# A fused attention, convolution and expert kernel: attention updates placed behind the next scores, and four smaller moves

## The chip, the cores and the metric

The kernel runs on one core of one Trainium2 chip. A core has a matrix engine (TensorE, PE in the profile), a vector engine (VectorE, DVE), a scalar engine (ScalarE, ACT), a general engine (GpSimd, POOL) and a queue engine (SyncE, SP) that here only issues transfers. Each engine works through its own list of instructions in order and waits on semaphores for the others. The metric is the device time of one execution in microseconds; lower is better.

## The reference

Three layers in a row, everything in float32. The core of it:

```python
# 1: decayed linear attention, B=2, H=8 heads, S=768, D=64; gamma differs per head
for t in range(S):
    state = gamma * state + einsum('bhd,bhe->bhde', k[:, :, t], v[:, :, t])
    y[:, :, t] = scale * einsum('bhd,bhde->bhe', q[:, :, t], state)
# 2: x = y as (2, 768, 512);  w_in 512x1024, conv_w 3x1024, w_out 1024x512
h = maximum(x @ w_in, 0)
conv_out = sum of conv_w[k] * (h shifted by k - 1 in the sequence), k = 0..2
x = (h * sigmoid(conv_out)) @ w_out
# 3: 8 experts, w1 512x1024, w2 1024x512
logits = x @ w_gate;  local_gate = sigmoid(x @ w_local)
e = argmax(logits[s]) if s == 0 or local_gate[s] < 0.5 else the expert of s - 1
out[s] = softmax(logits[s])[e] * (maximum(x[s] @ w1[e], 0) @ w2[e])
```

## The kernel before

**Precision.** Products that must be exact are made of three: a float32 matrix is split into a high part (a cast by ScalarE) and a low part (the value less its high part, by VectorE or GpSimd), and `three` (L961 to L963) multiplies high by low, low by high and high by high.

**Attention.** The 16 heads of both batches are taken as 8 pairs, i = 0 to 7. A pair's sequence is cut into 6 chunks of 128, in two halves g = 0, 1 of three chunks. For each pair TensorE makes: `scores(i, g)` (L991, keys times queries within chunks), `updates(i)` (L975, what each chunk adds to the state, into one bank), and `values(i, g)` (L1012 masked scores times values, L1009 scaled queries times state). VectorE makes `mask(i, g)` (scores times decay, L711), `scan(i)` (the states of all chunks from the updates, L697) and `y_lo(i, g)` (low part of the result, L718). ScalarE scales the keys that the updates read (`k_scale`, L531), two pairs ahead, and copies the results' high parts (L543). GpSimd scales the queries (L410). SyncE loads queries and keys for the scores (`qk`, 768 KB a pair), keys and values in rows (`kv`, 2 x 384 KB) and the decay tables (192 KB for each of the four pairs of heads). There are four buffers each for `qk` and `kv`; pair i + 4 is loaded once the values of pair i are done (`pv_done`). Behind them SyncE loads w_in in four pieces and, last, the output weights transposed and straight (2 MB each).

The weights of the input projection are split while the last pairs run: ScalarE casts four pieces (L547), GpSimd makes their four low parts (`lo`, L396). The convolution stage then starts with a gate product (`gate_first`, L1040, reads the transposed output weights), and its projection takes the four pieces one after another in its first sweep.

**Experts.** Tokens are sorted by expert into blocks of 128 (17 here, each of one expert). A block's rows are gathered from DRAM (`x2_rows`) by an indirect transfer from GpSimd, turned by TensorE (`turn_x`, L1214), split into `xT` high (ScalarE L625) and low (VectorE L891), multiplied by W1 (`through_w1`), passed through ReLU (ScalarE L620), turned (`turn_h`, L1262), split into `hT` high (L632) and low (L899) and multiplied by W2 (`through_w2`). VectorE scales the result (`evac_out`, L905), and GpSimd scatters it to the output (`scatter`, L449). An expert's weights come in 4 pieces of 128x1024 for W1 and 4 for W2; ScalarE casts each (L570), and the low parts are split between VectorE (L882) and GpSimd (L426). TensorE runs one block's W1 ahead of the previous block's W2.

Block 0 is special: its xT is made in two halves (ScalarE L650, VectorE L922), partly from rows that are still in SBUF. Block 1 is the first that needs `x2_rows` whole, with its last tile, which ScalarE writes in two halves (L648). Where a high and a low part are named in a list as `weights_lo(w, e, slot, pieces)`, w is 0 for W1 and 1 for W2, and e the expert.

The order on each engine is that of the code; no scheduler changes it.

## Time and profile before

| | us |
|---|---|
| median of 3 runs | 433.14 |
| lowest, highest | 432.61, 433.22 |
| the profiled execution | 432.46 |
| its span (first to last instruction) | 430.7 |
| TensorE busy in it | 413.1 |
| VectorE, ScalarE, GpSimd busy | 223.1, 196.0, 149.6 |

The profile is of one execution. Busy times are sums over instructions, and an engine that is not on the path may be idle without cost. In rows in order of time the first number is the start, the second the duration of the group in us, and the bracket at the end says how long the engine had been idle before it and whom it waited for.

### The profile page before, as it was taken

To read this page: it belongs to the slowest core of one execution; us is meant where nothing else is said; L and a number is where in the kernel's file an instruction comes from. 1 tells how busy PE (TensorE), PEld (TensorE's weight loads), DVE (VectorE), ACT (ScalarE), POOL (GpSimd) and SP (SyncE) were. 2 spreads that over 40 slices of the span, in tenths; PEclk is the share of its full clock that TensorE was granted. 3 is DMA by queue.
4 is the path that set the end of the run, shared out by engine and by line. 5 is a ranking of instruction groups with operands and counts; after the bars stand their busy time and mean duration, and the time that the engine had idled before them with its cause. 6 is when DMAs were issued, how large, how long until landed. Compare 5 with 4: busy or idle time off the path is not lost.

```text
span 430.7 us, 7239 instructions
## 1 busy us (share of the span) xinstructions
PE 413.1 (96%) x2641; PEld 349.0 (81%) x2642; DVE 223.1 (52%) x290; ACT 196.0 (46%) x276; POOL 149.6 (35%) x125
## 2 busy tenths in 40 slices
PE   7699999999999999999889999999999999999992
PEld 4588889987889987779778888888888888888862
DVE  4478837875002879389785422117642461726340
ACT  2244566862114666280435522128751472827440
POOL 3440884000000000015562821124882282653661
PEclk9999999999999999999999999999999999999997
DMA  8989900000321006742149391110479108366110
GB/s 299 414 336 372 420 22 2 0 2 0 148 97 49 2 0 258 328 148 97 50 157 419 132 410 52 49 50 24 173 278 414 67 25 330 128 229 235 36 33 9
DMA packets 15578, 67.77 MB, mean 157 GB/s; under 512 B 2559, under 2 KB 3583, under 8 KB 11200
## 3 DMA queue, kind: packets, MB, share of 16 engines
q1 hardware_dynamic: 12352, 58.88, 34.8%
q0 software_dynamic: 2912, 8.13, 5.8%
q8 instruction: 17, 0.28, 0.3%
q10 hardware_dynamic: 288, 0.41, 0.3%
q14 instruction: 9, 0.07, 0.1%
HBM read 58.49 MB, written 10.22 MB: 160 GB/s over the span
## 4 chain that ended last, share of the span: by engine, by line
PE 84%; DMA 5%; DVE 4%; ACT 2%; POOL 2%; SPq 1%; issue 1%; POOLq 0%; DVEq 0%
PE ps L961 24%; PE ps L963 23%; PE ps L962 23%; DMA kv<-qkv 5%; DVE wx L882 3%; PE ps L1262 3%; PE ps L1214 2%; PE ps L1012 1%; PE ps L1062 1%; PE ps L1009 1%; PE ps L991 1%; ACT wx L570 1%; POOL wx L426 1%; PE ps L975 1%; PE ps L1071 1%
## 5 line engine op out<-in xcount | busy, mean ns | idle before, releaser
L426 POOL TENSOR_TENSOR wx<-raw_w,wx 128x1024 fp32r<-128x1024 f32 x21 | 53.5, 2563 | 14.7 <-ACT wx L570 14.6
L961 PE MATMUL ps<-wx,xT 128*128 128x512 f32 x136 | 54.7, 402 | 2.4 <-DVE xT L891 1.5
L570 ACT CAST wx<-raw_w 128x1024 fp32r<-128x1024 f32 x56 | 54.8, 1057 | 1.9 <-issue 1.3
L961 PE MATMUL ps<-wx,hT 128*128 128x512 f32 x136 | 54.6, 401 | 0.7 <-POOL wx L426 0.7
L963 PE MATMUL ps<-wx,hT 128*128 128x512 f32 x136 | 53.1, 391 | 0.0
L963 PE MATMUL ps<-wx,xT 128*128 128x512 f32 x136 | 53.1, 391 | 0.0
L962 PE MATMUL ps<-wx,xT 128*128 128x512 f32 x136 | 53.0, 389 | 0.0
L962 PE MATMUL ps<-wx,hT 128*128 128x512 f32 x136 | 52.9, 389 | 0.0
L882 DVE TENSOR_TENSOR wx<-raw_w,wx 128x1024 fp32r<-128x1024 f32 x35 | 48.0, 1419 | 4.8 <-ACT wx L570 4.0
L632 ACT CAST hT<-ps 128x512 fp32r<-128x512 f32 x34 | 18.3, 590 | 57.1 <-PE ps L1262 57.1
L470 POOL TENSOR_TENSOR bk<-ge 128x240 f32<-128x240 f32 x1 | 0.6, 587 | 123.0 <-DVE ge L843 123.0
L961 PE MATMUL ps<-x,win 128*128 128x384 f32 x128 | 43.2, 337 | 0.0
L963 PE MATMUL ps<-x,win 128*128 128x384 f32 x128 | 42.8, 334 | 0.0
L962 PE MATMUL ps<-x,win 128*128 128x384 f32 x128 | 42.8, 334 | 0.0
L905 DVE TENSOR_SCALAR os<-ps,pslot 128x512 f32<-128x512 f32 x17 | 12.8, 751 | 57.1 <-PE ps L963 52.1
L620 ACT ACTIVATE hs<-ps 128x512 f32<-128x512 f32 x34 | 20.1, 597 | 46.1 <-PE ps L963 46.1
L961 PE MATMUL ps<-wout,hg 128*128 128x512 f32 (+1 forms) x104 | 40.1, 386 | 0.0
L891 DVE TENSOR_TENSOR xT<-ps,xT 128x512 fp32r<-128x512 f32 x17 | 11.7, 691 | 54.1 <-ACT xT L625 54.1
L962 PE MATMUL ps<-wout,hg 128*128 128x512 f32 (+1 forms) x104 | 38.9, 374 | 0.0
L963 PE MATMUL ps<-wout,hg 128*128 128x512 f32 (+1 forms) x104 | 38.9, 374 | 0.0
L750 DVE SCALAR_TENSOR_TENSOR cv<-hpad,cvw,cv 128x768 f32<-128x768 f32 x16 | 16.9, 1058 | 40.7 <-ACT cv L586 40.5
L449 POOL DMA_INDIRECT out<-os,snow x17 | 18.2, 1069 | 44.5 <-DVE os L905 32.9
(162 smaller groups left out, 813.3 us busy)
## 6 DMA issues: line engine op xcount, KB each, us to landing
raw_w<-w_exp SPq DMA_DIRECT2D x28, 1024.0 KB, 8.7
qk<-qkv SPq DMA_DIRECT2D x7, 768.0 KB, 7.4
...
```

The costliest lines, as they stand in the source:

```text
L426: ins = nc.gpsimd.tensor_tensor(wx[:, slot, 1, c], raw, wx[:, slot, 0, c].bitcast(F32), ALU.subtract)
L449: nc.gpsimd.indirect_dma_start(out_rows, bass.IndirectOffsetOnAxis(snow[:, 0:1], 0), os_[:], None, bounds_check=T - 1, oob_is_err=False).t ...
L570: nc.scalar.copy(wx[:, slot, 0, c], raw).then_inc(wx_hi[w], 1)
L620: nc.scalar.activation(hs[:, 512 * a:512 * a + 512], psP1[:, 512 * a:512 * a + 512], ACT.Relu).then_inc(h_done, 1)
L632: nc.scalar.copy(hT[:, 0, 4 * a:4 * a + 4, :].rearrange("p k t -> p (k t)"), psHT[:, 512 * a:512 * a + 512]).then_inc(hT_hi, 1)
L750: nc.vector.scalar_tensor_tensor(c[:], hp[:, 0:S], cvw[:, f, 0:1], c[:], ALU.mult, ALU.add).then_inc(tap0, 1)
L882: ins = nc.vector.tensor_tensor(wx[:, slot, 1, c], raw, wx[:, slot, 0, c].bitcast(F32), ALU.subtract)
L905: nc.vector.tensor_scalar(os_[:], psO, pslot[:, bass.ds(g, 1)], None, ALU.mult).then_inc(o_done, 1)
L961: mm(o, lh, rl, start=first, stop=False)
L962: mm(o, ll, rh, start=False, stop=False)
L963: return mm(o, lh, rh, start=False, stop=last)
L1262: last = nc.tensor.transpose(psHT[:, P * k:P * k + P], hs[:, P * k:P * k + P], ident)
```

## The change

Names and places are those of the code above.

- SyncE: pairs 1 to 3 are loaded alike, `qk`, keys, values, and each pair's decay table by itself: for pair 1 ahead of the values as before, for pairs 2 and 3 behind them. Keys and values of pairs 2 and 3 are two transfers now, with a semaphore each. The decay tables of pairs 2 and 3 were one transfer ahead of pair 2's `kv`.
- TensorE: `updates(i + 1)` stands between `scores(i + 1, 0)` and `values(i, 1)` for all pairs; it stood ahead of `values(i, 0)` for all but the first.
- ScalarE: `k_scale(i + 2)` follows the two copies of pair i; it preceded them. VectorE: `mask(i, 0)` precedes `scan(i)`.
- GpSimd: the low parts of w_in start one pair later: part 0 behind the scaling of pair 6, parts 1 to 3 behind that of pair 7.
- The last tile's rows are stored in two halves. GpSimd copies block 1's index before it waits for the stores, not after.
- VectorE at the start of the experts: first half of xT ahead of W2's piece 3; pieces 1 and 2 of expert 1's W1 behind block 0's hT.
- The last product waits for the four low parts of the last W2 in steps: VectorE's two at its start, GpSimd's ahead of its fifth and seventh groups; 4 filler matmuls ahead of it instead of 8. The last scatter's index is copied ahead of the wait for VectorE's result, which has a semaphore of its own.

```diff
@@ -325,21 +327,21 @@
             sp.dma_start(kv[0][:, 1, :], qkv[0, :, 3, :]).then_inc(kv_in[0], 16)
             sp.dma_start(decay[:, 0], decay_c[:, 0]).then_inc(decay0_in, 16)
             sp.dma_start(qk[0][:, :, HALF:S], qkv[0, :, 0:2, HALF:S]).then_inc(qk_in[0], 16)
-            sp.dma_start(qk[1][:], qkv[1, :, 0:2, :]).then_inc(qk_in[1], 16)
-            sp.dma_start(kv[1][:, 0, :], qkv[1, :, 2, :]).then_inc(k1_in, 16)
-            sp.dma_start(decay[:, 1], decay_c[:, 1]).then_inc(decay1_in, 16)
-            sp.dma_start(kv[1][:, 1, :], qkv[1, :, 3, :]).then_inc(kv_in[1], 16)
-            for i in range(2, B * NP_):
+            for i in range(1, NP_):
+                sp.dma_start(qk[i][:], qkv[i, :, 0:2, :]).then_inc(qk_in[i], 16)
+                sp.dma_start(kv[i][:, 0, :], qkv[i, :, 2, :]).then_inc(k_in[i], 16)
+                if i == 1:
+                    sp.dma_start(decay[:, i], decay_c[:, i]).then_inc(decay_in[i], 16)
+                sp.dma_start(kv[i][:, 1, :], qkv[i, :, 3, :]).then_inc(kv_in[i], 16)
+                if i > 1:
+                    sp.dma_start(decay[:, i], decay_c[:, i]).then_inc(decay_in[i], 16)
+            for i in range(NP_, B * NP_):
                 j = i % 4
-                if i >= 4:
-                    sp.wait_ge(pv_done, 2 * (i - 4) + 2)
+                sp.wait_ge(pv_done, 2 * (i - 4) + 2)
                 sp.dma_start(qk[j][:], qkv[i, :, 0:2, :]).then_inc(qk_in[j], 16)
-                if i == 2:
-                    sp.dma_start(decay[:, 2:], decay_c[:, 2:]).then_inc(decay_in, 16)
                 sp.dma_start(kv[j][:], qkv[i, :, 2:4, :]).then_inc(kv_in[j], 16)
-                if i >= 4:
-                    c = slice(1024 * (i - 4), 1024 * (i - 4) + 1024)
-                    sp.dma_start(win_raw[:, c], w_in[:, c]).then_inc(win_in[i - 4], 16)
+                c = slice(1024 * (i - 4), 1024 * (i - 4) + 1024)
+                sp.dma_start(win_raw[:, c], w_in[:, c]).then_inc(win_in[i - 4], 16)
                 if i == 5:
                     sp.dma_start(con[:], const_c).then_inc(const_in, 16)
             sp.dma_start(cvw[:], conv_w).then_inc(small_in, 16)
@@ -362,10 +364,16 @@
...
-                sp.wait_ge(x2_out, t + 1 if t < TT - 1 else TT + 1)
+                if t == TT - 1:
+                    break
+                sp.wait_ge(x2_out, t + 1)
                 if t < TT - 2:
                     sp.dma_start(x2_early[t * P:(t + 1) * P, :], x2n[:, t % 3, :]).then_inc(x2_stored[t % 3], 16)
                 sp.dma_start(x2_rows[t * P:(t + 1) * P, :], x2n[:, t % 3, :]).then_inc(x2_stored[t % 3], 16)
+            for n in range(2):
+                h = slice(DM // 2 * n, DM // 2 * n + DM // 2)
+                sp.wait_ge(x2_out, TT + n)
+                sp.dma_start(x2_rows[T - P:T, h], x2n[:, (TT - 1) % 3, h]).then_inc(x2_stored[(TT - 1) % 3], 16)
@@ -401,18 +409,15 @@
...
-                    pool.wait_ge(decay0_in, 16)
-                if i == 1:
-                    pool.wait_ge(decay1_in, 16)
-                if i == 2:
-                    pool.wait_ge(decay_in, 16)
+                if i < NP_:
+                    pool.wait_ge(decay_in[i], 16)
...
-                if i >= 5:
-                    lo(win, win_raw, i - 5)
-            for n in range(3, 4):
+                if i >= 6:
+                    lo(win, win_raw, i - 6)
+            for n in range(2, 4):
                 lo(win, win_raw, n)
@@ -426,7 +431,7 @@
...
-                        ins.then_inc(w2_last_lo if is_last(e) else w2_lo, 1)
+                        ins.then_inc(w2_last_lo_pool if is_last(e) else w2_lo, 1)
@@ -485,10 +490,15 @@
                 bounds_check=T - 2 * P - 1, oob_is_err=False).then_inc(gathered, 16)
             weights_lo(0, 0, 0, (3,))
             weights_lo(1, 0, 0, (0,))
+            pool.wait_ge(gathered, 16)
+            pool.wait_ge(xg_free, 2)
+            nc.gpsimd.tensor_copy(gnow[:], gidx[:, 1:2]).then_inc(g_copied, 1)
+            pool.wait_ge(g_copied, 2)
+            pool.sem_inc(rows_known, 1)
             for j in range(3):
-                pool.wait_ge(x2_stored[j], 32 * (TT // 3) - 16 * (j > 0))
-            pool.wait_ge(gathered, 16)
-            gather(1)
+                pool.wait_ge(x2_stored[j], 32 * (TT // 3) - 16 * (j == 1))
+            nc.gpsimd.indirect_dma_start(
+                xg[:], None, x2_rows, bass.IndirectOffsetOnAxis(gnow[:, 0:1], 0)).then_inc(gathered, 16)
             weights_lo(1, 0, 0, (1,))
@@ -510,7 +520,14 @@
             weights_lo(1, E - 1, 1, (2, 3))
             scatter(last)
             last = plain(E - 1)
-            scatter(last)
+            pool.wait_ge(scattered, 16 * last + 16)
+            nc.gpsimd.tensor_copy(snow[:], sidx[:, bass.ds(last, 1)]).then_inc(s_copied, 1)
+            pool.wait_ge(s_copied, last + 1)
+            pool.sem_inc(rows_known, 1)
+            pool.wait_ge(o_last, 1)
+            nc.gpsimd.indirect_dma_start(
+                out_rows, bass.IndirectOffsetOnAxis(snow[:, 0:1], 0), os_[:], None,
+                bounds_check=T - 1, oob_is_err=False).then_inc(scattered, 16)
             pool.wait_ge(gathered, 16 * last + 48)
             pool.wait_ge(scattered, 16 * last + 32)
@@ -525,7 +542,7 @@
...
-                act.wait_ge(k0_in if i == 0 else k1_in if i == 1 else kv_in[j], 16 * (i // 4 + 1))
+                act.wait_ge(k_in[i] if i < 4 else kv_in[j], 16 * (i // 4 + 1))
@@ -535,12 +552,12 @@
             k_scale(1)
             for i in range(B * NP_):
                 b, p = i // NP_, i % NP_
-                if i + 2 < B * NP_:
-                    k_scale(i + 2)
                 for g in range(2):
                     n, tb = 2 * i + g, S * b + HALF * g
                     act.wait_ge(pv_done, n + 1)
                     nc.scalar.copy(x1[:, 0, p, tb:tb + HALF], psY[n % 3]).then_inc(yhi_done, 1)
+                if i + 2 < B * NP_:
+                    k_scale(i + 2)
                 for n in {4: (0,), 5: (1, 2), 6: (3,)}.get(i, ()):
@@ -722,8 +736,8 @@
             scan(0)
             mask(0, 1)
             for i in range(1, B * NP_):
+                mask(i, 0)
                 scan(i)
-                mask(i, 0)
                 y_lo(i - 1, 0)
                 mask(i, 1)
                 y_lo(i - 1, 1)
@@ -899,10 +913,10 @@
...
+            def evac_out(g, done):
                 dve.wait_ge(p2_done, g + 1)
                 dve.wait_ge(scattered, 16 * g + 16)
-                nc.vector.tensor_scalar(os_[:], psO, pslot[:, bass.ds(g, 1)], None, ALU.mult).then_inc(o_done, 1)
+                nc.vector.tensor_scalar(os_[:], psO, pslot[:, bass.ds(g, 1)], None, ALU.mult).then_inc(done, 1)
@@ -910,22 +924,23 @@
...
             dve.wait_ge(tables, 1)
             weights_lo(0, 0, 0, (0, 1, 2))
-            weights_lo(1, 0, 0, (3,))
             for n in range(2):
+                if n == 1:
+                    weights_lo(1, 0, 0, (3,))
                 dve.wait_ge(x0_hi if n == 0 else xT_hi, 1)
                 nc.vector.tensor_tensor(xT[:, 1, 2 * n:2 * n + 2], psX0[:, 2 * n:2 * n + 2],
                                         xT[:, 0, 2 * n:2 * n + 2].bitcast(F32),
                                         ALU.subtract).then_inc(x0_lo if n == 0 else xT_done, 1)
-            weights_lo(0, 1, 1, (0, 1), True)
+            weights_lo(0, 1, 1, (0,), True)
             x_lo(1)
             h_lo(0)
-            weights_lo(0, 1, 1, (2,))
+            weights_lo(0, 1, 1, (1, 2))
...
             h_lo(last + 1)
             last = plain(E - 1)
-            evac_out(last)
+            evac_out(last, o_last)
@@ -967,7 +982,7 @@
                 pe.wait_ge(k_scaled, 2 * i + 2)
                 if i:
                     pe.wait_ge(st_done, 2 * i)
-                if i < 2:
+                if i < 4:
                     pe.wait_ge(kv_in[i], 16)
@@ -1020,13 +1035,10 @@
             warm_up(2, psY[2])
             pe.wait_ge(zeroed, 2)
             for i in range(B * NP_):
-                if 0 < i and i + 1 < B * NP_:
-                    updates(i + 1)
                 values(i, 0)
                 if i + 1 < B * NP_:
                     scores(i + 1, 0)
-                if i == 0:
-                    updates(1)
+                    updates(i + 1)
                 values(i, 1)
                 if i + 1 < B * NP_:
                     scores(i + 1, 1)
@@ -1241,11 +1253,13 @@
 
             def through_w2(g, e, slot):
                 if is_last(e):
-                    pe.wait_ge(w2_last_lo, 4)
+                    pe.wait_ge(w2_last_lo, 2)
                 else:
                     pe.wait_ge(w2_lo, 4 * e + 4)
                 pe.wait_ge(o_done, g + 1)
                 for k in range(KF):
+                    if is_last(e) and k in (4, 6):
+                        pe.wait_ge(w2_last_lo_pool, k // 2 - 1)
                     if k % 4 == 0:
                         pe.wait_ge(hT_done, 2 * g + k // 4 + 1)
@@ -1305,7 +1319,7 @@
             pe.wait_ge(w1_lo_dve, E)
             step(last_block, E - 2, 0, 1)
             last_block = plain(E - 1, 1)
-            warm_up(8, bank(7))
+            warm_up(4, bank(7))
             through_w2(last_block, E - 1, 1)
```

TensorE around pair 2's updates. In the rows kv_63 is pair 2's keys and values, kv_62 pair 1's, qk_59 pair 2's queries and keys; L975 are updates, L1009 and L1012 values, L991 scores. Before:

```order
L975 MATMUL ps<-kv_63 64x64 [waits st_done,k_scaled]
L975 MATMUL ps<-kv_63 64x64 x9
L1012 MATMUL ps<-probs_69,kv_62 64x128 [waits masked,q_scaled]
L1012 MATMUL ps<-probs_69,kv_62 64x128
L1009 MATMUL ps<-qs_66,state_72 64x128 [waits st_done]
L1009 MATMUL ps<-qs_66,state_72 64x128
L1012 MATMUL ps<-probs_69,kv_62 64x128 x2
L1009 MATMUL ps<-qs_66,state_72 64x128 x2
L1012 MATMUL ps<-probs_69,kv_62 64x128 x2
L991 MATMUL ps<-qk_59 128x128 [waits masked,qk_in2]
L991 MATMUL ps<-qk_59 128x128 x5
```

The same place now (L990 updates, L1024 and L1027 values, L1006 scores):

```order
L1027 MATMUL ps<-probs_69,kv_62 64x128 [waits masked,q_scaled]
L1027 MATMUL ps<-probs_69,kv_62 64x128
L1024 MATMUL ps<-qs_66,state_72 64x128 [waits st_done]
L1024 MATMUL ps<-qs_66,state_72 64x128
L1027 MATMUL ps<-probs_69,kv_62 64x128 x2
L1024 MATMUL ps<-qs_66,state_72 64x128 x2
L1027 MATMUL ps<-probs_69,kv_62 64x128 x2
L1006 MATMUL ps<-qk_59 128x128 [waits masked,qk_in2]
L1006 MATMUL ps<-qk_59 128x128 x5
L990 MATMUL ps<-kv_63 64x64 [waits kv_in2,st_done,k_scaled]
L990 MATMUL ps<-kv_63 64x64 x9
```

The updates that wait for pair 2's keys stood ahead of pair 1's first values and pair 2's first scores, and stand behind both now.

VectorE at the start of the experts, from W2's piece 3 (raw_first_94) and the two halves of block 0's xT (128x256) to block 0's hT; raw_w_1_96 is expert 1's W1. Before:

```order
L882 TENSOR_TENSOR wx<-raw_first_93,wx 128x1024 [waits wx_hi0] x2
L882 TENSOR_TENSOR wx<-raw_first_94,wx 128x1024 [waits wx_hi1]
L922 TENSOR_TENSOR xT<-ps,xT 128x256 [waits x0_hi]
L922 TENSOR_TENSOR xT<-ps,xT 128x256 [waits xT_hi]
L882 TENSOR_TENSOR wx<-raw_w_1_96,wx 128x1024 [waits wx_hi0] x2
L891 TENSOR_TENSOR xT<-ps,xT 128x512 [waits xT_hi]
L899 TENSOR_TENSOR hT<-ps,hT 128x512 [waits hT_hi] x2
L882 TENSOR_TENSOR wx<-raw_w_1_96,wx 128x1024 [waits wx_hi0]
```

Now (L896 weights, L937 and L905 xT, L913 hT):

```order
L896 TENSOR_TENSOR wx<-raw_first_93,wx 128x1024 [waits wx_hi0] x2
L937 TENSOR_TENSOR xT<-ps,xT 128x256 [waits x0_hi]
L896 TENSOR_TENSOR wx<-raw_first_94,wx 128x1024 [waits wx_hi1]
L937 TENSOR_TENSOR xT<-ps,xT 128x256 [waits xT_hi]
L896 TENSOR_TENSOR wx<-raw_w_1_96,wx 128x1024 [waits wx_hi0]
L905 TENSOR_TENSOR xT<-ps,xT 128x512 [waits xT_hi]
L913 TENSOR_TENSOR hT<-ps,hT 128x512 [waits hT_hi] x2
L896 TENSOR_TENSOR wx<-raw_w_1_96,wx 128x1024 [waits wx_hi0] x2
```

The first half of xT went ahead of W2's piece 3, and one of two pieces of expert 1's W1 went behind block 0's hT.

GpSimd at the same place, the second gather. Before:

```order
L426 TENSOR_TENSOR wx<-raw_first_93,wx 128x1024 [waits wx_hi0]
L426 TENSOR_TENSOR wx<-raw_first_94,wx 128x1024 [waits wx_hi1]
L436 CAST gnow<-gidx 128x1 [waits gathered,x2_stored2,xg_free,x2_stored1,x2_stored0]
L439 DMA xg<-x_rows,gnow 128x512 [waits g_copied]
L426 TENSOR_TENSOR wx<-raw_first_94,wx 128x1024 [waits wx_hi1]
L436 CAST gnow<-gidx 128x1 [waits xg_free,gathered,tables]
```

Now (L431 weights, L495 and L500 the second gather):

```order
L431 TENSOR_TENSOR wx<-raw_first_93,wx 128x1024 [waits wx_hi0]
L431 TENSOR_TENSOR wx<-raw_first_94,wx 128x1024 [waits wx_hi1]
L495 CAST gnow<-gidx 128x1 [waits xg_free,gathered]
L500 DMA xg<-x_rows,gnow 128x512 [waits g_copied,x2_stored2,x2_stored1,x2_stored0]
L431 TENSOR_TENSOR wx<-raw_first_94,wx 128x1024 [waits wx_hi1]
L441 CAST gnow<-gidx 128x1 [waits xg_free,gathered,tables]
```

The index copy no longer waits for the stores (x2_stored); the transfer behind it does.

## Rows read from the trace of the kernel before

**Rows 1.** The page, part 1: busy us (share of the span) xinstructions.

```profile
PE 413.1 (96%) x2641; PEld 349.0 (81%) x2642; DVE 223.1 (52%) x290; ACT 196.0 (46%) x276; POOL 149.6 (35%) x125
```

**Rows 2.** TensorE in order of time: start us, us, line, operation [wait <-for whom].

```profile
14.85 0.94 PE L991 MATMUL ps<-qk 64*128 64x128 f32 x12
...
19.63 1.19 PE L975 MATMUL ps<-kv 128*64 128x64 f32 x20 [3.85 <-ACT kv L531]
...
23.92 0.50 PE L1009 MATMUL ps<-qs,state 128*64 128x128 f32 x4
...
26.32 0.80 PE L975 MATMUL ps<-kv 128*64 128x64 f32 x20
...
31.43 0.80 PE L975 MATMUL ps<-kv 128*64 128x64 f32 x20
...
54.66 1.92 PE L1040 MATMUL ps<-woutT,wgl 128*32 128x512 f32 x16
```

**Rows 3.** Stretches: us; busy us of PE, PEld, DVE, ACT, POOL; PEclk, DMA share, GB/s.

```profile
20.00:23.00 3.00, 3.00 (x38) 2.67 (x34) 2.97 (x5) 1.09 (x3) 1.83 (x1) 0.50 1.02 418
28.00:33.00 5.00, 5.00 (x91) 4.43 (x88) 4.27 (x7) 2.08 (x4) 1.81 (x1) 1.00 1.03 419
25.20:27.40 2.20, 2.20 (x48) 1.91 (x46) 1.28 (x3) 1.54 (x3) 0.78 (x1) 1.00 0.42 95
```

**Rows 4.** ScalarE in order of time, attention.

```profile
18.46 1.12 ACT L531 ACTIVATE kv<-kv,con 128x384 f32<-128x384 f32 x2 [6.18 <-DMA kv<-qkv]
...
44.94 1.12 ACT L531 ACTIVATE kv<-kv,con 128x384 f32<-128x384 f32 x2 [2.60 <-DMA kv<-qkv]
```

**Rows 5.** The load queue (SyncE) in order of time: the issue after pair 1.

```profile
25.55 0.33 SPq L336 DMA_DIRECT2D qk<-qkv  x1
```

**Rows 6.** GpSimd in order of time, end of the attention.

```profile
50.14 1.82 POOL L410 TENSOR_TENSOR qs<-qk,decay 128x768 f32<-128x768 f32 x1
51.93 4.72 POOL L396 TENSOR_TENSOR win<-win_raw,win 128x1024 fp32r<-128x1024 f32 x2
```

**Rows 7.** TensorE in order of time, start of the experts.

```profile
208.70 0.47 PE L961 MATMUL ps<-wx,xT 128*128 128x512 f32 x1 [0.86 <-DVE xT L922]
...
218.33 0.49 PE L961 MATMUL ps<-wx,xT 128*128 128x512 f32 x1 [1.50 <-DVE xT L891]
```

**Rows 8.** ScalarE in order of time, start of the experts.

```profile
207.16 0.37 ACT L650 CAST xT<-ps 128x256 fp32r<-128x256 f32 x1 [3.93 <-PE ps L1145]
...
211.05 3.89 ACT L570 CAST wx<-raw_w 128x1024 fp32r<-128x1024 f32 x4
...
215.99 0.59 ACT L625 CAST xT<-ps 128x512 fp32r<-128x512 f32 x1
```

**Rows 9.** VectorE in order of time, start of the experts.

```profile
212.13 4.13 DVE L882 TENSOR_TENSOR wx<-raw_w,wx 128x1024 fp32r<-128x1024 f32 x1 [0.53 <-ACT wx L570]
...
217.32 0.68 DVE L891 TENSOR_TENSOR xT<-ps,xT 128x512 fp32r<-128x512 f32 x1
```

**Rows 10.** GpSimd in order of time, start of the experts.

```profile
210.75 0.18 POOL L436 CAST gnow<-gidx 128x1 uint32<-128x1 f32 x1 [3.62 <-DMA x_rows<-x2n]
211.74 1.00 POOL L439 DMA_INDIRECT xg<-x_rows,gnow  x1 [0.81 <-POOL gnow L436]
```

**Rows 11.** TensorE in order of time, the end.

```profile
414.61 1.89 PE L954 MATMUL ps<-warm 128*128 128x512 bf16 x8
417.24 0.49 PE L961 MATMUL ps<-wx,hT 128*128 128x512 f32 x1 [0.74 <-POOL wx L426]
```

**Rows 12.** VectorE in order of time, the end.

```profile
415.04 1.29 DVE L899 TENSOR_TENSOR hT<-ps,hT 128x512 fp32r<-128x512 f32 x2
...
423.21 0.75 DVE L905 TENSOR_SCALAR os<-ps,pslot 128x512 f32<-128x512 f32 x1 [6.88 <-PE ps L963]
```

**Rows 13.** GpSimd in order of time, the end.

```profile
421.64 0.18 POOL L445 CAST snow<-sidx 128x1 uint32 x1 [2.59 <-DMA out<-os,snow]
424.96 1.00 POOL L449 DMA_INDIRECT out<-os,snow  x1 [3.13 <-DVE os L905]
```

22 lines of the change are left out of this document (10 added, 12 removed).

## Prediction

> **What bounds the kernel.** I first read the span and the engines' busy shares: TensorE is busy for 413.1 of 430.7 us [rows 1], so only some 17 us are not its work, and its order of time says where they lie. Beside the start and the tail, in which the result leaves, there are four places where it stands: 3.85 us before the state updates of pair 2 [rows 2], 0.86 and 1.50 us at the start of the experts [rows 7], and 0.74 us, plus a filler, before the last product [rows 11]. The change touches all four. I then read who is waited for there. At 19.63 TensorE waits for ScalarE's scaling of pair 2's keys, which starts at 18.46 when the load of keys and values has landed [rows 2, 4]. After the wait it also runs slower: between 20 and 23 us the granted clock is 0.50, that is 1.2 instead of 2.4 GHz; it had stood still from 15.8 to 19.6 us [rows 2, 3]. The loads run at some 419 GB/s, but at 25.2 to 27.4 us their queue is nearly empty (95 GB/s), because pair 5's loads are issued only at 25.55, when pair 1's last values are done [rows 3, 5].
>
> **Attention, the order on TensorE.** No matmul is added or removed. Before, `updates(2)` stands ahead of `values(1, 0)` and `scores(2, 0)`; now it stands behind them. At 15.8 us both have what they need: pair 1's scan ended before, with the masks and the queries, and pair 2's queries and keys for the scores came ahead of the second stretch of keys and values. At the full clock, updates, first values and first scores of a pair take together 5.11 (26.32 to 31.43) less 2.40 (23.92 to 26.32, the second halves), so 2.71 us [rows 2]. Of these the updates are about 0.8 at most by their own row, so TensorE comes to them at about 15.85 + 2.71 - 0.7 = 17.9.
> Are the keys there? Before they land at 18.43. The third transfer of decay tables (384 KB for pairs 2 and 3) went ahead of them; now pair 2's own 192 KB goes behind its values. 384 KB at 419 GB/s are 0.94 us, so the values land at about 17.5; the keys, now a transfer of their own of 384 KB, another 0.94 earlier, at 16.6. ScalarE has put its copies ahead of the scaling (`pv_done` 2 comes before the scores of 14.85) and is free; the two scalings take 1.12 [rows 4] and end at 17.7. So the wait is 0 to 0.5 us, I take 0.1. The second values then start at 15.85 + 2.71 + 0.1 = 18.66 instead of 23.92 [rows 2]: 5.26 us gained, 3.7 of it the wait and 1.6 the stretch at 1.2 GHz (4.29 us from 19.63 to 23.92 for the work of 2.71).
>
> **What is late next.** After that TensorE's pace is 5.11 us a pair, as before. VectorE's order changes with it (the mask before the scan), and its work of a pair fits: 4.27 busy in 5 us [rows 3]. The scan now has the second values and second scores, 2.4 us, as its cover; mask and scan need about 2.0 after the updates. GpSimd's query scaling of pair 2 needs the decay table that lands behind the values, at 18.0, and is due at about 21: covered.
> The loads are nearer. TensorE comes to `updates(7)` at 17.9 + 0.1 + 5 x 5.11 = 43.6. Before, those keys landed at 44.9 and were scaled at 46.06 [rows 4]. They come earlier, since pair 5's loads are issued once the second values of pair 1 are done, at about 18.66 + 1.5 (2.40 less the 0.94 of scores) = 20.2, instead of at 25.55: the hole of 2.2 us at 95 GB/s, worth 1.7 us, closes, and the later pairs' loads too are queued well before the queue is empty. That makes 43.2 at the latest (scaled 44.4, a wait of 0.8); if the slow stretches at each restart of the queue go as well, 41.8 (scaled 42.9, no wait). I take 0.4 us of wait, in between. The attention stage then gives 5.26 - 0.4 = 4.9 us; bounds 2.8 (landing not earlier at all: 46.06 against 43.6 is a wait of 2.46) and 5.3.
> Everything behind it must come along. The weights' low parts: before, query scaling 7 (50.14) stood behind low part 1, and two parts followed it until 56.65 [rows 6]. Now scaling 7 goes first and three parts of 2.36 follow, from about 44 to 51.5; the fourth is due when the gate's first product (1.9 us from 49.8) and three quarters of the input projection's first sweep are over, at about 53.3 (both estimates). Covered by 1.8. If ScalarE's casts, which wait behind the scaling of pair 7, were 2 us later, it would cost 0.2.
>
> **Start of the experts.** On VectorE the low part of W2's piece 3 stood ahead of the first half of xT; TensorE waited 0.86 for that half until 208.70 [rows 7]. Its high part was ready at 207.53 [rows 8]. Moved ahead, the half is ready about 0.55 us earlier, and TensorE with it; the rest of the 0.86 is the way over ScalarE. All that hangs on TensorE there moves by 0.55: ScalarE's four casts (211.05), the ReLUs behind them and the high part of block 1 (215.99) [rows 8].
> On GpSimd the index copy now precedes the wait for the stores. Before, 210.75 (store landed) to 211.74 (gather issued) are 0.99 us [rows 10]; now the gather is issued at 210.8, about 0.9 us earlier, and lands before the ReLUs end. It isn't what decides, since ScalarE is busy until 215.4. On VectorE one weight piece instead of two stands ahead of block 1's low part, which began at 217.32 although its input was ready at 216.58 (215.99 + 0.59) [rows 8, 9]: 0.7 us. Together 0.55 + 0.7 = 1.25 us at 218.33; bounds 0.5 (the piece still in the way) and 1.6. The two pieces now behind the hT halves are due only where the second expert starts, a block of 12 us later: nothing.
> The Trainium skill, "SBUF — State Buffer", section "SBUF: two separate sides", says that a VectorE operation with two SBUF inputs and a GpSimd operation that reads SBUF shut each other out for a whole instruction. The piece that began at 212.13 took 4.13 us, across the gather's issue (211.74 to 212.74) and the weight piece that follows it on GpSimd [rows 9, 10]; by the page a gather's issue alone would not hold it, by the row it did. By the page the piece would be through at 212.8 in the new order, by the row at about 215.2; both are ahead of 216.0, so the sum stays.
>
> **The end.** The last product waited for all four low parts of the last W2, the last from GpSimd, and started at 417.24 [rows 11]. Now it starts with VectorE's two parts and takes GpSimd's before its fifth and seventh group. Four fillers end at about 415.6 (eight took 1.89); the first hT half is ready at 415.04 + 0.65 = 415.7 [rows 12]. I take a start at 415.9: 1.3 us. GpSimd's last part is due at the seventh of eight groups, 415.9 + 6 x 0.75 ((423.21 - 417.24) / 8) = 420.4, and there before 417.24. Of the last scatter, 1.0 us lay between VectorE's end (423.21 + 0.75) and its issue at 424.96 [rows 12, 13]; the copy of the index and the message are now ahead of the wait. Something between 0 and 1.0 goes; 0.4. The copy can't start before 421.64 (previous scatter) [rows 13], which leaves about 1 us until VectorE's new end at 422.65: just enough. End: 1.7 us; bounds 1.1 and 2.3.
>
> **The sum.** 4.9 + 1.25 + 1.7 = 7.85 us. The profiled execution took 432.46 us (span 430.7), so 424.6; against the median of 433.14 it is 425.3, which I predict. The bounds of the terms give 4.4 to 9.2 us of gain, so 423.9 to 428.7.
>
> **Rivals.**
> A, the loads take over: TensorE runs up to keys that land nearly as before. For it: their queue is at 419 GB/s outside the hole. Against: the hole itself and the earlier releases. With 46.06 unmoved the attention gives 2.8, in all 5.75: 427.4. Chance 0.15.
> B, the start of the experts is held on as before: the single piece waits for GpSimd twice, or the gather lands late. For it: 4.13 us for one piece, and GpSimd's pieces in a row. Against: 0.7 us of room. 1.25 becomes 0.5: 426.0. Chance 0.15.
> C, slower: TensorE's clock. If the new order leaves short waits in each pair (masks, scans, loads), the clock could stay at 1.2 GHz through the attention. The rows price it: 4.29 us for 2.71 of work, 1.58 times as long, so 3.0 us more a pair; from the third pair in a row on it outweighs the 7.85 gained, and over six pairs it gives 433.1 - 7.85 + 18 = 443. The skill ("TensorE: Matmul & The Clock Gate", Part 1) says the clock follows how busy the engine has been. Against it: before, the clock is at 1.00 wherever TensorE works without a long gap [rows 3], and the new order has fewer gaps. Chance 0.03.
> D, it doesn't do what it says: what is gained up to 50 us is taken back at a later meeting, the transposed output weights (2 MB, the last but one load) or the low parts of the input weights. The loads all follow the same queue, which still has 2 MB after them. Then some 3 us of the attention are lost, in all about 428.5 to 430. Chance 0.06.
> My forecast, with its neighbours, has 0.61.
>
> **Chances.** About 0.2% (0.9 us) can be told from no change. A, B and the forecast are all faster, D too. So faster 0.95, same 0.02, slower 0.03. The range for 8 in 10: 424.0 to 428.5.
>
> **What would show it.** In the new profile: no wait over 0.6 us before pair 2's updates and no stretch at 0.50 before 50 us; pair 2's keys scaled by 17.7; the gate's first product at 49.8 (50 to 52 is rival A); no hole in the loads before the last one; block 1's first product 1.25 us closer behind block 0's than the stage's shift explains (from there to the end TensorE unchanged); the last product 0.2 us behind hT's first half, and the last scatter issued 0.6 us after VectorE. I am wrong if TensorE waits at `updates(6)` or `updates(7)` for over 1 us, or if VectorE's reordered scan becomes what values wait for.

## The result and the profile after

The changed kernel takes 425.52 us (median of 4 runs, 424.74 to 426.35); the kernel before, timed beside it, 432.88 us (4 runs, 431.25 to 433.22). The ratio is 0.9838, 95% interval 0.9806 to 0.9869. Predicted were 425.3 us, range 424.0 to 428.5. The profiled execution took 425.42 us, its span is 423.7.

The total hides one step that did not come. Five marks on TensorE's and GpSimd's path, in both traces, split the 7.05 us:

| mark | before | after | earlier by | newly gained | predicted |
|---|---|---|---|---|---|
| gate's first product | 54.66 | 49.03 | 5.63 | 5.63 | 4.9 |
| block 0's first W1 product | 208.70 | 202.48 | 6.22 | 0.59 | 0.55 |
| block 1's first W1 product | 218.33 | 212.85 | 5.48 | -0.74 | 0.7 |
| last expert's first W2 product | 417.24 | 410.34 | 6.90 | 1.42 | 1.3 |
| last scatter issued | 424.96 | 417.91 | 7.05 | 0.15 | 0.4 |

The page after, part 1: TensorE is busy 3.2 us less than in [rows 1] although it does the same products. No stretch of the attention runs at half clock now, which is 1.6 us of it (see fill_the_wait), and there are 4 fillers fewer, by estimate 0.9 us (eight took 1.89, [rows 11]); the rest was not traced.

```profile
PE 409.9 (97%) x2636; PEld 346.6 (82%) x2638; DVE 220.1 (52%) x290; ACT 196.2 (46%) x276; POOL 150.8 (36%) x125
```

TensorE in order of time in the attention (updates of pairs 1, 2, 3 and 7, the gate's first product). They answer to [rows 2]: no row has a bracket, the wait of 3.85 us is gone, and the updates stand 5.11 us apart from pair 1 to pair 7.

```profile
12.60 0.80 PE L990 MATMUL ps<-kv 128*64 128x64 f32 x20
...
17.71 0.80 PE L990 MATMUL ps<-kv 128*64 128x64 f32 x20
...
22.82 0.80 PE L990 MATMUL ps<-kv 128*64 128x64 f32 x20
...
43.24 0.80 PE L990 MATMUL ps<-kv 128*64 128x64 f32 x20
...
49.03 1.49 PE L1052 MATMUL ps<-woutT,wgl 128*32 128x512 f32 x12
```

The stretches of [rows 3] after the change (columns as there): granted clock 1.00 where it was 0.50, and 423 GB/s where the load queue had been nearly empty at 95.

```profile
20.00:23.00 3.00, 3.00 (x50) 2.59 (x52) 2.31 (x5) 1.90 (x4) 0.28 (x1) 1.00 1.05 419
25.20:27.40 2.20, 2.20 (x38) 1.91 (x38) 2.17 (x4) 1.35 (x4) 1.13 (x1) 1.00 1.04 423
```

ScalarE's scalings of pairs 2 and 7, the answer to [rows 4]. Both come about 3 us earlier; pair 7's ends at 43.15, just ahead of the updates of 43.24.

```profile
15.36 1.12 ACT L548 ACTIVATE kv<-kv,con 128x384 f32<-128x384 f32 x2
...
42.03 1.12 ACT L548 ACTIVATE kv<-kv,con 128x384 f32<-128x384 f32 x2 [1.19 <-DMA kv<-qkv]
```

The start of the experts, TensorE (answers to [rows 7]). The wait before block 0 fell from 0.86 to 0.30, but the one before the turn of block 1's rows grew from 0.46 to 1.84 us: their gather has not landed.

```profile
202.48 0.47 PE L976 MATMUL ps<-wx,xT 128*128 128x512 f32 x1 [0.30 <-DVE xT L937]
...
210.46 0.66 PE L1226 MATMUL ps<-con,xg 128*128 128x128 f32 x4 [1.84 <-DMA xg<-x_rows,gnow]
210.96 1.04 PE L1276 MATMUL ps<-con,hs 128*128 128x128 f32 x8
212.85 0.49 PE L976 MATMUL ps<-wx,xT 128*128 128x512 f32 x1 [0.86 <-DVE xT L905]
```

The same place on ScalarE, VectorE and GpSimd (answers to [rows 8 to 10]). ScalarE, busy until 209.70, now waits 1.45 for the turn, VectorE 4.63 for ScalarE. GpSimd stood still for 4.90 until 206.49, as the store of the last rows landed only at 205.70, and the gather's issue took 1.53 instead of 1.00 beside VectorE's piece of 205.92.

```profile
208.62 1.08 ACT L637 ACTIVATE hs<-ps 128x512 f32<-128x512 f32 x2
211.16 0.59 ACT L642 CAST xT<-ps 128x512 fp32r<-128x512 f32 x1 [1.45 <-PE ps L1226]
```

```profile
205.92 1.23 DVE L896 TENSOR_TENSOR wx<-raw_w,wx 128x1024 fp32r<-128x1024 f32 x1 [0.53 <-ACT wx L587]
211.77 0.69 DVE L905 TENSOR_TENSOR xT<-ps,xT 128x512 fp32r<-128x512 f32 x1 [4.63 <-ACT xT L642]
```

```profile
206.49 1.53 POOL L500 DMA_INDIRECT xg<-x_rows,gnow  x1 [4.90 <-DMA x_rows<-x2n]
```

The end, TensorE, VectorE, GpSimd (answers to [rows 11 to 13]). The last product starts 0.09 us behind hT's first half (409.60 + 0.65); the scatter is issued 0.84 us behind VectorE's end (417.07), where it was 1.00. The index was copied ahead of that result before, too (421.64 against 423.96, [rows 12, 13]); what is newly ahead of the wait is only GpSimd's message that the rows are known.

```profile
410.34 0.50 PE L976 MATMUL ps<-wx,hT 128*128 128x512 f32 x1 [0.15 <-DVE hT L913]
```

```profile
409.60 1.29 DVE L913 TENSOR_TENSOR hT<-ps,hT 128x512 fp32r<-128x512 f32 x2
416.32 0.75 DVE L919 TENSOR_SCALAR os<-ps,pslot 128x512 f32<-128x512 f32 x1 [5.44 <-PE ps L978]
```

```profile
415.94 0.18 POOL L524 CAST snow<-sidx 128x1 uint32 x1 [2.31 <-DMA out<-os,snow]
417.91 0.99 POOL L528 DMA_INDIRECT out<-os,snow  x1 [1.78 <-DVE os L919]
```

### The profile page after: what moved, and what is told of

Same layout as the page of the kernel before. It is cut to its first block, busy times and chain, and to the rows that moved or that the text cites. A ratio compares the mean times of both kernels' runs of the same rounds, so it can differ in the third digit from the quotient of the medians.

```text
span 423.7 us, 7234 instructions
## 1 busy us (share of the span) xinstructions
PE 409.9 (97%) x2636; PEld 346.6 (82%) x2638; DVE 220.1 (52%) x290; ACT 196.2 (46%) x276; POOL 150.8 (36%) x125
## 4 chain that ended last, share of the span: by engine, by line
PE 93%; DMA 3%; DVE 1%; ACT 1%; issue 1%; POOL 0%; ACTq 0%; POOLq 0%; DVEq 0%
PE ps L976 25%; PE ps L978 25%; PE ps L977 25%; PE ps L1276 3%; PE ps L1006 3%; PE ps L1027 3%; PE ps L1024 2%; PE ps L1226 2%; PE ps L990 1%; PE ps L1074 1%; DMA kv<-qkv 1%; DMA xg<-x_rows,gnow 1%; DMA x_rows<-x2n 1%; PE ps L1083 1%; PE ps L1052 0%
## 5 line engine op out<-in xcount | busy, mean ns | idle before, releaser
L431 POOL TENSOR_TENSOR wx<-raw_w,wx 128x1024 fp32r<-128x1024 f32 x21 | 53.6, 2565 | 14.7 <-ACT wx L587 14.6
L978 PE MATMUL ps<-wx,xT 128*128 128x512 f32 x136 | 53.1, 391 | 0.0
L978 PE MATMUL ps<-wx,hT 128*128 128x512 f32 x136 | 53.1, 391 | 0.0
L896 DVE TENSOR_TENSOR wx<-raw_w,wx 128x1024 fp32r<-128x1024 f32 x35 | 45.8, 1355 | 4.6 <-ACT wx L587 3.9
L905 DVE TENSOR_TENSOR xT<-ps,xT 128x512 fp32r<-128x512 f32 x17 | 11.7, 691 | 57.6 <-ACT xT L642 57.6
L764 DVE SCALAR_TENSOR_TENSOR cv<-hpad,cvw,cv 128x768 f32<-128x768 f32 x16 | 18.3, 1145 | 39.4 <-ACT cv L603 39.3
L454 POOL DMA_INDIRECT out<-os,snow x16 | 17.2, 1073 | 40.6 <-DVE os L919 29.9
```

The source lines that it names most:

```text
L431: ins = nc.gpsimd.tensor_tensor(wx[:, slot, 1, c], raw, wx[:, slot, 0, c].bitcast(F32), ALU.subtract)
L454: nc.gpsimd.indirect_dma_start(out_rows, bass.IndirectOffsetOnAxis(snow[:, 0:1], 0), os_[:], None, bounds_check=T - 1, oob_is_err=False).t ...
L764: nc.vector.scalar_tensor_tensor(c[:], hp[:, 0:S], cvw[:, f, 0:1], c[:], ALU.mult, ALU.add).then_inc(tap0, 1)
L896: ins = nc.vector.tensor_tensor(wx[:, slot, 1, c], raw, wx[:, slot, 0, c].bitcast(F32), ALU.subtract)
L978: return mm(o, lh, rh, start=False, stop=last)
```

## Experiments: the three parts apart

**attn_only**: the kernel before with the first four points of the change (loads, order on TensorE, ScalarE and VectorE, GpSimd's low parts), nothing behind the attention. Of its diff:

```diff
@@ GpSimd
-                if i >= 5:
-                    lo(win, win_raw, i - 5)
+                if i >= 6:
+                    lo(win, win_raw, i - 6)
@@ VectorE
+                mask(i, 0)
                 scan(i)
-                mask(i, 0)
```

> The kernel before with the attention parts of the change alone: loads, order of updates, key scaling behind the copies, mask ahead of scan, low parts of w_in one pair later. My theory: this is where nearly all of the gain lies. The gate's first product comes at 49.0 us instead of 54.66, nothing behind it changes, so the time is 5.6 us less: 427.3, ratio 0.987. Rival (the three sites help each other): under 5 us alone, the rest only together with the other parts.

Measured: 427.69 us, ratio 0.9881 (0.9863 to 0.9898); gate's first product at 49.91, and the marks follow it at the old distances within 0.1 us: block 0 at 203.91, block 1 at 213.51, last W2 product at 412.40. So the attention gives 4.8 us of the 7.0 in this run, whose start happened to be 0.9 us later (updates of pair 1 at 13.47 instead of 12.60).

**end_only**: the kernel before with the last point of the change alone. Of its diff:

```diff
-                    pe.wait_ge(w2_last_lo, 4)
+                    pe.wait_ge(w2_last_lo, 2)
...
-            warm_up(8, bank(7))
+            warm_up(4, bank(7))
```

> The kernel before with the parts of the change at the end alone. Theory: last product 1.4 us earlier (415.8 instead of 417.24), last scatter 1.55 us earlier, time 1.5 us less (ratio 0.9965). Rival (previous scatter still holds the last result): last scatter under 1 us earlier.

Measured: 431.51 us, ratio 0.9966 (0.9941 to 0.9990); the last expert's first W2 product is at 415.81, 1.43 us earlier, with block 1's first product where it was (218.40); the last scatter at 423.39, 1.57 earlier. The term of the end is real and is not hidden.

**experts_only**: the kernel before with the store in halves, the early index copy and VectorE's order. Of its diff:

```diff
@@ VectorE
-            weights_lo(1, 0, 0, (3,))
             for n in range(2):
+                if n == 1:
+                    weights_lo(1, 0, 0, (3,))
...
-            weights_lo(0, 1, 1, (0, 1), True)
+            weights_lo(0, 1, 1, (0,), True)
```

> The kernel before with the parts of the change at the start of the experts alone. Theory F (an instruction fetch of 16 KB, which comes at a fixed point of TensorE's program, now meets the store of the last tile on one of the 16 transfer engines): block 0's first product 0.55 us earlier, the second half's store lands over 3 us after its issue, with one engine over 1 us behind the others, and block 1's first product is not earlier than 218.1: time as before, ratio 0.998 to 1.001. Rival L (only VectorE's weight piece, which holds GpSimd off, delays the gather): the store lands within 2 us, block 1's product at 217.6 or earlier, 0.7 us gained. Rival M (my prediction): 1.25 us gained.

Measured: 432.97 us, ratio 0.9997 (0.9978 to 1.0016): nothing. Block 0's first product comes 0.57 us earlier behind the gate's, block 1's 0.15 later (163.82 against 163.67 us behind it), with nearly the changed kernel's wait for the gather, 1.81 us. The three parts' gains, 1.19, 0.34 and 0.03%, make 1.56% of the whole's 1.62%.

## Experiments: inside the attention

**loads_only**: the first point of the change (SyncE) alone. Of its diff:

```diff
-                if i == 2:
-                    sp.dma_start(decay[:, 2:], decay_c[:, 2:]).then_inc(decay_in, 16)
-                sp.dma_start(kv[j][:], qkv[i, :, 2:4, :]).then_inc(kv_in[j], 16)
...
+                sp.dma_start(kv[i][:, 0, :], qkv[i, :, 2, :]).then_inc(k_in[i], 16)
...
+                sp.dma_start(kv[i][:, 1, :], qkv[i, :, 3, :]).then_inc(kv_in[i], 16)
...
+                sp.dma_start(decay[:, i], decay_c[:, i]).then_inc(decay_in[i], 16)
```

> The kernel before with the loads of the change alone (keys and values of pairs 2 and 3 apart, their decay tables behind them). Theory (the loads carry most): pair 2's keys land at 15.3 and values at 16.3, its updates start at about 16.5 instead of 19.63, no stretch at 0.50, and later pair 7's keys cost some 1 us: gate's first product at 50.3 to 51.5, 3.2 to 4.3 us gained. Rival (the loads alone are worth the 0.94 us of the decay table): 53.7.

Measured: 429.62 us, ratio 0.9917 (0.9887 to 0.9948); the wait before pair 2's updates falls from 3.85 to 0.90 us and no stretch is at 0.50, but the gate's first product is at 51.91, slightly later than expected. TensorE in order of time in this kernel, pairs 2, 4 and 6 and the last queries: with the updates ahead of the values, it comes just too early for the keys again and again.

```profile
16.95 0.80 PE L970 MATMUL ps<-kv 128*64 128x64 f32 x20 [0.90 <-ACT kv L529]
...
27.73 0.80 PE L970 MATMUL ps<-kv 128*64 128x64 f32 x20 [0.29 <-ACT kv L529]
...
38.31 0.80 PE L970 MATMUL ps<-kv 128*64 128x64 f32 x20 [0.28 <-ACT kv L529]
...
49.32 0.44 PE L1007 MATMUL ps<-probs,kv 128*64 128x128 f32 x4 [0.50 <-POOL qs L408]
```

**pe_order_only**: TensorE's new order alone.

```diff
-                if 0 < i and i + 1 < B * NP_:
-                    updates(i + 1)
                 values(i, 0)
                 if i + 1 < B * NP_:
                     scores(i + 1, 0)
-                if i == 0:
-                    updates(1)
+                    updates(i + 1)
```

> The kernel before with TensorE's order of the change alone (updates behind the next pair's first scores); loads, ScalarE, VectorE and GpSimd as before. Theory (the order is of little worth without the others): pair 2's keys still land at 18.4, ScalarE's copies stand behind their scaling and VectorE's second mask behind those, so pair 1's second values start at about 21.4 (23.92 before, 18.4 after), and each later pair waits some 0.3 us for the mask that now stands behind the scan: gate's first product 52 to 53.5, 1 to 2.5 us gained. Rival (the order is the gain): 50 or earlier.

This was a miss: 434.08 us, ratio 1.0036 (1.0005 to 1.0066), 0.4% slower where a gain was expected. TensorE, updates of pair 4, its first values and updates of pair 5: the pace is 5.80 us a pair, not 5.11, and 0.60 of it is a wait for VectorE's mask.

```profile
33.20 0.80 PE L975 MATMUL ps<-kv 128*64 128x64 f32 x20
36.86 0.44 PE L1012 MATMUL ps<-probs,kv 128*64 128x128 f32 x4 [0.60 <-DVE probs L711]
39.00 0.80 PE L975 MATMUL ps<-kv 128*64 128x64 f32 x20
```

VectorE in the same kernel: the scan waits for the updates, and the mask, whose scores are older, starts only when the scan has ended and has no wait of its own.

```profile
28.25 1.67 DVE L697 TENSOR_TENSOR_SCAN state<-gpow,ps 64x320 f32<-64x320 f32 x2 [1.43 <-PE ps L975]
29.95 0.96 DVE L711 TENSOR_TENSOR probs<-ps,decay 128x768 f32<-128x768 f32 x1
```

**pe_dve_act_order**: the same with the mask ahead of the scan and the scaling behind the copies, loads as before.

```diff
@@ VectorE, beside the edit above
+                mask(i, 0)
                 scan(i)
-                mask(i, 0)
```

> The kernel before with the new order of the attention on TensorE, VectorE (mask ahead of scan) and ScalarE (scaling behind the copies), with the old loads and GpSimd's old order. Theory: what made TensorE's order alone slower was that VectorE's mask stood behind the scan that the later updates had delayed, 0.6 us a pair. With the mask first the pace is 5.11 us a pair again; pair 2's updates wait for its keys to about 19.6, and the last pair's for keys that land near 44.9, so the gate's first product is at 51.0 to 52.3 and the median at 429.5 to 430.8. Rival: the pace is lost to the order on TensorE itself (scan and second mask have too little between updates and second values): 5.8 us a pair stays, gate's first product about 57, 434.

Measured: 431.25 us (7 runs, 428.66 to 431.99), ratio 0.9948 (0.9919 to 0.9977). The updates of pairs 3 to 6 are 5.11 apart again (26.29, 31.40, 36.51, 41.61), so the pace wasn't lost to TensorE's order itself. That it was the mask, and not ScalarE's scaling, which moved with it, is read from the rows above; no run moves the mask alone. The gate's first product, 53.38, is 1.1 us later than the latest that was expected: pair 2's updates still wait for the keys (1.85, until 19.64), the clock is 0.51 from 20.2 to 23.6, and near 45 us TensorE waits 0.78 for GpSimd's query scaling, which here still stands behind a low part. The fourth point of the change, which moves the low parts, was not tried alone; this wait and the 0.50 in loads_only are what the runs show for it. In time, by the ratios on some 432.9 us: TensorE's order alone loses 1.6 us, the order on all three engines gains 2.3, the loads alone 3.6, all of it 5.2. The gains don't add up: the same wait and the same slow stretch can be saved only once.

**fill_the_wait**: 16 filler matmuls in the wait of the kernel before, ahead of pair 2's updates, nothing else.

```diff
+                if i == 1:
+                    warm_up(16, psY[2])
                 if 0 < i and i + 1 < B * NP_:
                     updates(i + 1)
```

> The kernel before with 16 filler matmuls (384 columns) in TensorE's wait for pair 2's keys, nothing else. If 1.6 of the 5.3 us ahead of pair 1's second values are the clock: no stretch at 0.50 before the end, updates of pair 2 again at 19.63, but second values of pair 1 at 22.3 instead of 23.92, gate's first product at 53.1, 1.6 us gained. Rival: later meetings (pair 7's keys, which land at 44.9) take it back, gate's first product later than 53.8, under 0.9 us gained.

Measured: 431.10 us, ratio 0.9968 (0.9938 to 0.9997). The updates of pairs 2 and 3 are 5.11 us apart (19.78 and 24.89) where they were 6.69 (19.63 and 26.32): 1.58 us are the clock. The gate's first product is at 53.24, 1.42 earlier, near the 53.1 expected. The stretch 15 to 27 us of this kernel, columns as in [rows 3], has the clock at 1.00; the kernel before has 0.86 there.

```profile
15.00:27.00 12.00, 11.64 (x176) 9.29 (x174) 8.91 (x13) 4.85 (x10) 5.46 (x3) 1.00 1.01 392
```

## Experiments: the start of the experts

The store of the last rows took 3.1 us from issue to landing after the change. The records of the transfers in that stretch show one thing beside it: a fetch of instructions, 16 KB on one of the 16 engines that carry the store. In the trace fifteen of the store's sixteen parts have landed by 204.31 and the last one lands at 205.70; its packets start when the fetch (203.61 to 204.52) has ended. The DMA view of the changed kernel, 202 to 206 us (per queue packets, MB and share; issues with KB and us to landing):

```profile
q1 hardware_dynamic: 144, 0.13, 10.3%
q8 instruction: 1, 0.02, 1.4%
...
x_rows<-x2n SPq DMA_DIRECT2D x1, 128.0 KB, 3.1
```

**shift20**: the changed kernel with 20 fillers of 32 columns ahead of pair 0's updates, which should move the points at which TensorE's instructions are fetched.

```diff
             warm_up(6, psY[2])
+            warm_up(20, psY[2][:, 0:32])
             updates(0)
```

> The changed kernel with 20 filler matmuls of 32 columns in TensorE's wait ahead of the first updates (8.05), which put every fetch of TensorE's program 40 instructions earlier. Theory F (the fetch meets the last tile's store): the fetch now begins at 200 to 202 us, the second half's store lands at about 204.2 instead of 205.70, gather issued at 205.0, TensorE's turn of block 1 no longer waits 1.84 us but under 0.4, block 1's first product 1.2 to 1.5 us earlier (211.5): 424.1, ratio to the kernel before 0.979. Rival L (the lock with VectorE's piece and the gather's own time): store lands as late as before or the gather is as late, block 1's product at 212.4 or later, time as the changed kernel's.

Measured: 425.73 us, ratio 0.9825 (0.9788 to 0.9863). The fetch now starts at 199.79 instead of 203.61 and the one before it at 178.21 instead of 184.13, although the work comes 1.6 us later, so these fetches are TensorE's. The same view of this kernel, 203 to 207 us, has no fetch and a landing after 1.7 us:

```profile
q1 hardware_dynamic: 144, 0.13, 9.7%
...
x_rows<-x2n SPq DMA_DIRECT2D x1, 128.0 KB, 1.7
```

TensorE does not wait for the gather, and block 1 is 9.63 us behind block 0 instead of 10.37. The fillers cost 1.1 us at the updates of pair 0 (9.16, in the changed kernel 8.05) and 1.6 from those of pair 1 on (14.22 against 12.60), and take the gain back.

**no_piece**: the changed kernel with piece 0 of expert 1's W1 also behind hT on VectorE.

```diff
-            weights_lo(0, 1, 1, (0,), True)
...
-            weights_lo(0, 1, 1, (1, 2))
+            weights_lo(0, 1, 1, (0, 1, 2))
```

> The changed kernel with all three of VectorE's weight pieces of expert 1 behind block 0's hT, so that none runs beside the issue of block 1's gather. Theory: the issue takes 1.0 us instead of 1.53 and lands 0.5 us earlier, with the store as late as before (205.7); block 1's first product 0.5 us earlier (212.35). Rival F alone: the issue's length doesn't matter, product at 212.85.

Measured: 425.17 us, ratio 0.9820 (0.9772 to 0.9868). The gather's issue takes 1.00 us again, but the fetch had moved too (200.13), so this run does not price the piece alone. It also says that TensorE's program alone does not fix the time of a fetch: here that program is the changed kernel's, the fetch before lies at 184.36 as there (184.13), and this one still starts 3.5 us earlier. What else decides it is open, and since each kernel has one trace, so is how often a kernel's other executions meet it. The run's main use lies elsewhere: VectorE waits 4.82 us for xT's high part, its low part is done at 211.13, and block 1 starts only at 212.30.

**whole_store**: the changed kernel with the last rows stored in one transfer.

```diff
-            for n in range(2):
-                h = slice(DM // 2 * n, DM // 2 * n + DM // 2)
-                sp.wait_ge(x2_out, TT + n)
-                sp.dma_start(x2_rows[T - P:T, h], ...)
+            sp.wait_ge(x2_out, TT + 1)
+            sp.dma_start(x2_rows[T - P:T, :], ...)
```

> The changed kernel with the last tile's rows stored in one transfer again, once both halves are written. Theory F (an instruction fetch of TensorE lies on one of the store's engines): halves are not what makes the landing late; where a fetch starts within the store it lands about 3.1 to 3.4 us behind block 0's first W1 product and TensorE waits 1.8 to 2.3 us for block 1's rows; where none does it lands 1.6 to 2.2 behind it, TensorE does not wait and the two blocks' first products are 9.6 apart, which gives 424.6 to 425.0. Rival: the two half transfers are the slow thing (more descriptors of half the size): then the landing comes about 1 us earlier than in the changed kernel whether or not a fetch lies on it, 424.7.

Measured: 426.77 us (5 runs, 425.54 to 427.12), ratio 0.9849 (0.9821 to 0.9878). With the fetch on it the whole store lands after 3.9 us, later than the half, so it isn't the halves that make the landing slow.

Seven of the kernels side by side, in order of the fetch; "low part" is the end of xT's low part, the last columns are block 1's first product behind block 0's and behind the end of block 0's ReLU:

| kernel | fetch in the store | store, KB and us | wait for gather | ReLU end | low part | block 1 | behind block 0 | behind ReLU |
|---|---|---|---|---|---|---|---|---|
| whole_store | yes | 256, 3.9 | 2.16 | 210.15 | 213.22 | 213.61 | 10.70 | 3.46 |
| experts_only | yes | 128, 3.3 | 1.81 | 216.19 | 218.92 | 219.31 | 10.35 | 3.12 |
| changed | yes | 128, 3.1 | 1.84 | 209.70 | 212.46 | 212.85 | 10.37 | 3.15 |
| before | yes, late in it | 256, 2.3 | 0.46 | 215.93 | 218.00 | 218.33 | 9.63 | 2.40 |
| attn_only | no | 256, 2.0 | none | 211.14 | 212.98 | 213.51 | 9.60 | 2.37 |
| shift20 | no | 128, 1.7 | none | 211.35 | 212.55 | 213.75 | 9.63 | 2.40 |
| no_piece | no | 128, 1.7 | none | 209.93 | 211.13 | 212.30 | 9.59 | 2.37 |

Two things stand in it. Every landing with a fetch within the store is late (before only slightly: there the fetch starts at 210.00, as the store's packets end). And block 1 never starts less than 2.37 us behind the end of block 0's ReLU, however early the low part is (in no_piece 1.17 us earlier); in the five kernels that the table leaves out and that lack the edit below it is 2.39 to 2.41. So the piece that stood ahead of the low part before was not what held block 1: two chains met there within 0.1 us. What TensorE does in the 2.4 us is eight turns, the loading of two registers and the branches into the expert loop. That was tested:

**range_first** and **range_first_no_piece**: the changed kernel and no_piece with the register loads of expert 0's range between the two turns (the loop's first two experts written out).

```diff
             turn_x(1)
+            first, last_block = block_range(pe, 0)
             turn_h(0, False)
```

> The changed kernel with the register loads of expert 0's range placed ahead of the turn of block 0's ReLU result, all else as changed. Theory G: here xT's low part decides (its end plus 0.39 us) as long as the last rows' store is met by the fetch, so block 1's first product stays 10.3 to 10.4 us behind block 0's and the median is that of the changed kernel, 425.2 to 425.8. If the fetch has moved off the store, the two products are 8.8 to 9.4 apart and the median is 424.3 to 425.0. Rival H: 10.4 or 9.6 apart, never below 9.6.

> The changed kernel, with the low part of piece 0 of expert 1's W1 behind hT like pieces 1 and 2, and on TensorE the two registers that give expert 0's range of blocks loaded between the turns of block 1's rows and of block 0's ReLU result, where they were loaded behind both at the entry of the expert loop (whose first two experts are written out for it); nothing computed differs. Theory G: in all kernels so far block 1's first product came 2.37 to 2.40 us behind the end of block 0's ReLU, or 0.39 us behind xT's low part if that was later; the 2.4 us are TensorE's eight turns and the register loads and branches of the loop's entry. Taken out of it, the 2.4 fall to about 1.6, where the low part (1.20 behind ReLU) decides: block 1's first product 8.8 us behind block 0's first instead of 9.6, median 424.3 to 424.8 if the store of the last rows meets no instruction fetch. If a fetch meets it: 10.0 to 10.4 between the two products, about 425.3. Rival H: the 2.4 us are the way from ReLU's semaphore through the turns alone, or the matmul's own start; then 9.6 stays and the median is 425.2.

Measured: in range_first the fetch had moved (200.00), the store landed after 1.7 us, and block 1 starts at 211.08, 8.57 us behind block 0 and 1.34 behind ReLU. TensorE there:

```profile
208.66 0.66 PE L1226 MATMUL ps<-con,xg 128*128 128x128 f32 x4
210.17 1.09 PE L1276 MATMUL ps<-con,hs 128*128 128x128 f32 x8 [0.85 <-ACT hs L637]
211.08 0.49 PE L976 MATMUL ps<-wx,xT 128*128 128x512 f32 x1
```

So the registers' loading and the loop's entry, which this edit changes together, were the 1 us, and the profiled execution has the last W2 product at 408.51, 1.83 us earlier than the changed kernel, and took 423.6 us. But the median of 6 runs is 426.75 (423.6 to 428.3), ratio 0.9862 (0.9834 to 0.9889): no better. In the profiled run the mean granted clock is 0.994; in four of the other five it is 0.990 or 0.988, and they take 426.7 to 428.3. Where they lose it no trace shows. In range_first_no_piece the fetch met the store (it landed after 3.3 us), block 1 is 10.11 us behind block 0, within the 10.0 to 10.4 expected, and the median is 425.54, ratio 0.9836 (0.9807 to 0.9865). None of the variants beats the changed kernel by more than the intervals.

## Why the prediction was right, and where it was not

**Attention, 4.9 predicted, 5.63 measured.** Mechanism and size of the wait and the clock hold: the updates of pair 2 at 17.71 (17.9 forecast), 1.58 us by the clock (1.6). Of the 0.7 more, 0.5 come from the loads, which I took too late: the waits of 0.1 at pair 2's updates and of 0.4 at pair 7's did not come. Pair 2's keys were scaled from 15.36, so they had landed 1.2 us ahead of my 16.6, and pair 7's were scaled at 43.15. I had counted back from 18.43 as if the queue's pace had set it; in the trace before, fifteen of the sixteen parts of pair 2's keys and values had landed by 17.34, and the last came 1.1 us later, with a fetch of instructions beside it (16.22 to 17.32). Another 0.1 is chance at the start (updates of pair 1 at 12.60 against 12.71). The size is known no better than that: in the six profiles with this attention and no fillers added, the gate's first product lies at 49.03 to 49.91, in the three with the old one (before, end_only, experts_only) at 54.66 to 55.49; by their medians the attention gives 5.4. VectorE's new order, which I had only checked for room, matters too: TensorE's order with the old loads costs 2.5 us at the gate's first product without VectorE's and ScalarE's (57.12 against 54.66) and gains 1.3 with them (53.38). With the new loads this was not tried.

**Start of the experts, 1.25 predicted, -0.15 measured.** The first half, 0.55, came (0.59). The failed step is "on VectorE one weight piece instead of two stands ahead of block 1's low part ...: 0.7 us". I read the wait's name, VectorE's low part, and did not ask when TensorE itself would have been ready: 2.4 us behind ReLU, the very time at which it started before, and in no trace without range_first's edit earlier. The piece was worth nothing. The gather also became the bound, which I had excluded ("it isn't what decides"): a fetch of TensorE's instructions, which started as the store's packets ended before (0.91 us behind the first of them) and 0.18 us behind the first now, made the landing some 1.4 us late (3.1 against 1.7). Block 0's 0.6 us are most of that shift, but as no_piece shows, they are not all that sets a fetch's time. Rival B had the place ("the gather lands late") and not the cause; its price, 0.5 instead of 1.25, was still 0.65 above what came.

**The index copy, 0.9 predicted, 0.4 measured.** I took 210.75, the copy's start, for the store's landing [rows 10]. The last part had landed at 210.54, so from landing to issue it was 1.20 us, as in all seven profiles with the old order (within 0.01). With the copy ahead of the wait it is 0.79 (205.70 to 206.49), in all seven again. The rest can't go this way: behind its last wait GpSimd takes some 0.8 us until the issue of an indirect transfer starts. It is alike at the end, 0.16 gained for 0.4, where the copy had been ahead of the wait already.

**GpSimd and VectorE.** The Trainium skill, "SBUF — State Buffer", section "SBUF: two separate sides", says that of a VectorE operation with two SBUF inputs and a GpSimd operation that reads SBUF the one that starts first has the shared port pair for its whole length. The rows agree and go further, since they show it for a gather's issue: the piece of 205.92 was first and took 1.23 us, and the issue took 1.53 (in experts_only 1.32), ending 0.87 us behind the piece both times. In range_first the issue was first (205.11), and the piece of 205.95 took 3.69 us, until GpSimd's next piece (206.14, 2.41 us) had ended as well.

**The end, 1.7 predicted, 1.57 measured.** 1.42 and 0.15, for 1.3 and 0.4.

**The total.** 7.05 for 7.85: 0.7 more from the attention against 1.4 less from the experts. That the predicted time was met within 0.3 us is luck: two errors of opposite sign stood in it.
